# The tokens' factors computed earlier and with fewer steps, and expert products that wait for their weights piece by piece

## The reference

```
logits = x @ w_gate;  e_idx = argmax(logits, axis=1)
probs = exp(logits - logits.max(-1, keepdims=True))
probs /= probs.sum(-1, keepdims=True) + 1e-09
gate_w = probs[arange(N), e_idx]
eom = 1.0 / (1.0 + exp(-(x @ w_output_gate)))
for e in range(E):
    mask = e_idx == e
    h = maximum(x[mask] @ w1[e], 0.0)
    out[mask] = gate_w[mask, None] * eom[mask, e, None] * (h @ w2[e])
```

## Time and profile before

| | us |
|---|---|
| median of 3 runs | 1444.78 (1444.0 to 1448.49) |
| the profiled execution | 1446.43 |
| its span, first to last instruction | 1444.7 |
| busy: PE, DVE, ACT, POOL | 1358.1, 866.3, 621.3, 382.7 |

### The profile page before, as it was taken

The page is one execution under the profiler, slowest core; times in us unless marked ns, Lnnn a source line. Parts: engine busy times, 40 slices in busy tenths (PEclk is TensorE's granted clock), DMA queues, the critical chain, the costliest instruction groups (busy, mean ns, idle before and its releaser), DMA issues. The chain is left out here.

```text
span 1444.7 us, 24541 instructions
## 1 busy us (share of the span) xinstructions
PE 1358.1 (94%) x7653; PEld 1197.4 (83%) x7653; DVE 866.3 (60%) x1622; ACT 621.3 (43%) x1523; POOL 382.7 (26%) x307
## 2 busy tenths in 40 slices
PE   4999999999999999559979999989999999999998
PEld 3788888888888888447867888868999999999997
DVE  2899999999999998774434444436532323332232
ACT  3888888888888887311143011005411111111111
POOL 4122222222222235586498022023001010200000
PEclk9999999999999999769989999999999999999999
DMA  7755555556656664266366221016300000000000
GB/s 167 172 128 127 126 126 126 130 130 133 132 131 133 134 133 124 98 210 217 119 221 223 66 82 65 15 45 181 110 30 15 30 15 31 15 22 1 0 23 22
DMA packets 125343, 144.91 MB, mean 100 GB/s; under 512 B 48416, under 2 KB 91040, under 8 KB 123360
## 3 DMA queue, kind: packets, MB, share of 16 engines
q1 hardware_dynamic: 110192, 103.37, 29.2%
q10 hardware_dynamic: 11648, 29.36, 6.3%
q0 software_dynamic: 3440, 11.27, 2.7%
HBM read 84.48 MB, written 19.66 MB: 72 GB/s over the span
## 5 line engine op out<-in xcount | busy, mean ns | idle before, releaser
L637 ACT ACTIVATE p_hl<-ps_t 128x512 fp32r<-128x512 f32 (+1 forms) x336 | 196.0, 586 | 79.7 <-PE ps_t L812 77.5
L761 DVE TENSOR_TENSOR p_hl<-ps_t,p_hl 128x512 fp32r<-128x512 f32 (+1 forms) x336 | 217.4, 667 | 14.3 <-ACT p_hl L637 8.4
L893 PE MATMUL ps_o<-p_hl,v_hl 128*128 128x512 f32 x558 | 198.4, 436 | 0.0
L812 PE MATMUL ps_t<-ident,probs 128*128 128x128 f32 x1296 | 196.2, 273 | 0.8 <-DVE p_hl L761 0.4
L812 PEld LDWEIGHTS ps_t<-ident,probs 128*128 128x128 f32 x1296 | 160.0, 140 | 27.0 <-DVE p_hl L761 3.5
L653 ACT ACTIVATE probs<-ps_s_late,neg_max 128x384 f32<-128x384 f32 x288 | 165.2, 578 | 28.3 <-DVE neg_max L704 26.3
L1714 ACT ACTIVATE silu<-ps_g 128x384 f32<-128x384 f32 x72 | 35.4, 492 | 315.8 <-PE ps_g L1820 315.7
L927 PE MATMUL ps_s_late<-kq_t 128*128 128x384 f32 x640 | 159.8, 360 | 9.1 <-ACT probs L653 7.7
L1767 DVE TENSOR_TENSOR silu<-ps_g,silu 128x384 f32<-128x384 f32 x72 | 40.1, 558 | 212.0 <-ACT silu L1714 212.0
L1139 POOL TENSOR_TENSOR w_parts<-raw_w,w_parts 128x1024 fp32r<-128x1024 f32 x56 | 132.0, 2395 | 99.7 <-ACT w_parts L1207 99.7
L1207 ACT ACTIVATE w_parts<-raw_w 128x1024 fp32r<-128x1024 f32 x56 | 58.5, 1058 | 220.4 <-POOL w_parts L1139 97.7
(11 more groups left out here) (202 smaller groups left out, 2862.2 us busy)
## 6 DMA issues: line engine op xcount, KB each, us to landing
raw_w<-in_moe_w ACTq DMA_DIRECT2D x56, 512.0 KB, 4.1
kq_t<-kept_rows SPq DMA_DIRECT2D x30, 608.0 KB, 6.3
kq_t<-kept_rows SPq DMA_DIRECT2D x32, 320.0 KB, 7.1
raw_k<-in_k SPq DMA_DIRECT2D x32, 288.0 KB, 5.6
raw_v<-in_v SPq DMA_DIRECT2D x16, 576.0 KB, 4.8
kq_t<-kept_rows SPq DMA_DIRECT2D x30, 288.0 KB, 6.6
raw_q<-in_q SPq DMA_DIRECT2D x32, 256.0 KB, 4.1
y_by_slot<-x_out SPq DMA_DIRECT2D x25, 256.0 KB
```

Source lines behind the costliest of these rows:

```text
L637: nc.scalar.activation(p_hi[prob_ring(kind, m)][:, 0:w], T[ring(kind, j)][:, 0:w], ACT.Copy).then_inc(hi_ready, 1)
L761: nc.vector.tensor_tensor(p_lo[n][:, 0:w], t[:, 0:w], p_hi[n][:, 0:w].bitcast(F32), ALU.subtract).then_inc(t_free, 1)
L812: last = nc.tensor.transpose(dst[:, n * P:(n + 1) * P], src, ident[:, :])
L893: last = nc.tensor.matmul(sums_of(kind, what)[:, :], v_hl[v_par][:, c * P:(c + 1) * P], part[:, :], start=(i == 0 and n == 0), stop=(i == ...
```

## The change

Two edits, both in `route_and_experts`.

1. The chain of factors. The eleven DVE instructions become six. The numerator 1 is left out, and the two factors' denominators are multiplied before one reciprocal of 18 columns; of the 144-column operations one product and two reductions remain. The chain stands ahead of xs_parts(0) instead of behind it.
2. The waits for weights on PE. `up` waited for all four pieces of w1, then ran over the halves h and inside over the chunks c; now it runs over c, waits for piece c, and inside over h. `down` waited for all four pieces of w2; now it waits for one piece every two chunks. The matmuls are the same; both HB banks are filled in turn, and up_half is incremented for both at the last chunk.

```
+                dve.wait_ge(exp_out, 1)
+                link(nc.vector.tensor_tensor(big[2][:, :], big[3][:, :], onehot[:, :], ALU.mult))
+                nc.vector.reduce_sum(small[1][:, :], by_e(big[1]), AX)
+                link(nc.vector.reduce_sum(small[3][:, :], by_e(big[2]), AX))
+                link(nc.vector.tensor_scalar(small[3][:, :], small[3][:, :], 1.0, None, ALU.add))
+                link(nc.vector.scalar_tensor_tensor(out=small[2][:, :], in0=small[1][:, :], scalar=1e-9,
+                                                    in1=small[3][:, :], op0=ALU.add, op1=ALU.mult))
+                nc.vector.reciprocal(coef[:, :], small[2][:, :]).then_inc(coef_ready, 1)
+
                 xs_parts(0)
-
-                dve.wait_ge(exp_out, 1)
-                link(nc.vector.reduce_sum(small[1][:, :], by_e(big[1]), AX))
-                link(nc.vector.tensor_tensor(big[1][:, :], big[1][:, :], onehot[:, :], ALU.mult))
-                link(nc.vector.reduce_sum(small[0][:, :], by_e(big[1]), AX))
-                link(nc.vector.tensor_scalar(small[1][:, :], small[1][:, :], 1e-9, None, ALU.add))
-                link(nc.vector.reciprocal(small[2][:, :], small[1][:, :]))
-                link(nc.vector.tensor_scalar(big[3][:, :], big[3][:, :], 1.0, None, ALU.add))
-                link(nc.vector.reciprocal(big[2][:, :], big[3][:, :]))
-                link(nc.vector.tensor_tensor(big[2][:, :], big[2][:, :], onehot[:, :], ALU.mult))
-                link(nc.vector.reduce_sum(small[3][:, :], by_e(big[2]), AX))
-                link(nc.vector.tensor_tensor(small[0][:, :], small[0][:, :], small[2][:, :], ALU.mult))
-                nc.vector.tensor_tensor(coef[:, :], small[0][:, :], small[3][:, :], ALU.mult).then_inc(coef_ready, 1)
-
                 hidden(0)
...
-                    pe.wait_ge(w_ready[0], W1P * e + W1P)
                     pe.wait_ge(xst_ready, i + 1)
                     base = pe.snap((e % 2) * (2 * WCOLS))
-                    for h in range(FH):
-                        for c in range(DC):
+                    for c in range(DC):
+
+                        pe.wait_ge(w_ready[0], W1P * e + c + 1)
+                        for h in range(FH):
...
-                                                                    stop=(c == DC - 1))
-                        last.then_inc(up_half, 1)
+                                                    stop=(c == DC - 1))
+                            if c == DC - 1:
+                                last.then_inc(up_half, 1)
...
-                    pe.wait_ge(w_ready[1], W2P * e + W2P)
...
                     for c in range(FC):
+                        if c % (FC // W2P) == 0:
+
+                            pe.wait_ge(w_ready[1], W2P * e + c // (FC // W2P) + 1)
```

## The result

The changed kernel takes 1432.38 us (median, 1430.69 to 1434.58), beside 1444.88 for the kernel before on the same chip: a ratio of 0.9904, 95% interval 0.9884 to 0.9924, so 11 to 17 us less. The forecast was 1431, in a range of 1424 to 1437. The profiled execution took 1430.82 us, its span is 1429.0.

A forecast was written before the change was run, and what follows sets the result against it. From 775.9 us the kernel was taken as PE's row of matmuls, so only reaching that state earlier counts: 8.5 us (chain) plus 5.4 (pieces) is 13.9, giving 1431 us, range 1424 to 1437.

The forecast's parts named there:

- The chain, 12.6 us at tile 1: DVE before tile 0's parts: six instructions take 1.6 us in idle time, cost 0; tile 1 starts 12.6 us earlier.
- rival C: DVE's product meets POOL's residues in its new place, if started after 618.33: tile 1 7.5 us late, 1447 us; chance 0.04.
- the rest of a gather, 0.95 us: Chain in its new place beside POOL's gathers: the most that contention could cost, 0.95 us, still covered by idle time.
- What is late next: tile 0's store behind L1111: DVE's copy of tile 1 waits until 664.2 for a store in SP's queue; down(2) starts at 667.6, lead 10.1 us.
- G: Lead left after the store's wait and PE's low clock, carried through tile 5 to experts 4 and 5: 8.0 to 10.0, taken 8.5.
- delay up(3) by some 4 us inside this same wait: If DVE's nameless pause until 656.85 recurs, it delays tile 3's up product some 4 us within the store's wait, costing nothing else.
- ACT and POOL follow PE: Preparation of weights for experts 4 and 5 waits for tile 5's down product, so it moves earlier if tile 5 does.
- The pieces, 5.4 us: PE's up product at tile 9, waiting piece by piece, ends 4.7 to 5.9 us sooner; 5.4 taken.
- rival B: The pieces bring nothing, since PE's clock falls in the trickle and later waits eat the rest: 1436 us; chance 0.16.
- Two waits for the price of one: Tile 8's gain from the pieces, up to 6 us, does not add, because tile 9 waits for POOL again.
- 150 waits at nothing: Three more waits per up and per down product on PE, 150 in all, cost 0; other bound 16 us.
- The lock: DVE's two-SBUF-input product waits for all eight POOL residues, about 17 us, not one of 2.4 us as the skill page says.

The follow-up runs named there:

- e4: The changed kernel with the old long chain put ahead of tile 0's parts, moved but not shortened: 1447.89 us, ratio 1.0001 to the kernel before.
- e5: The changed kernel with the last tiles' rows saved from POOL's queue instead of SP's: 1423.44 us, ratio 0.9855 to the kernel before.
- e1: The kernel before with the new short chain ahead of tile 0's parts, PE's waits and loops as they were: 1440.66 us, ratio 0.9955.
- e8: The changed kernel itself, unaltered, run on the chip of e5 to e7: 1433.78 us, ratio 0.9929 to the kernel before.
- the first four experiments: e1 to e4, all on one chip, testing chain and pieces apart: ratios 0.9955, 0.9948, 1.0012 and 1.0001 to the kernel before.
- e2: The changed kernel with the old chain back behind tile 0's parts, so the waits by pieces alone: 1439.42 us, ratio 0.9948 to the kernel before.
- e7: The changed kernel with each of PE's waits for a piece issued four times, 600 waits more: 1433.35 us, ratio 0.9929 to the kernel before.
- e3: The kernel before with the new short chain left in the old place, behind tile 0's parts: 1449.83 us, ratio 1.0012.
- e11: e5 with weight preparation on ACT and POOL reordered, from expert 3 on, with expert 5's second weights ahead of expert 6's first: 1412.8 us, ratio 0.978.
- e6: e5 with eight of POOL's residues made between the gathers of kept rows and those of late rows: 1423.38 us, ratio 0.9855 to the kernel before.

## Why the prediction was right

*The chain, 12.6 us at tile 1.* Right: 12.8 us from t0. DVE's six instructions took 1.62 us where 1.6 stood, in idle time. Their safety was overrated: I put the point from which rival C decides at 618.33, 3.3 us after the chain's start, and reckoned contention only while a residue runs. In e4 a start 0.59 us before the first residue's row was already too late. Between the end of the last instruction with two SBUF inputs (L1385, 614.81) and POOL's residues (616.98) lie 2.2 us: that is the margin of this change, and a few instructions more would eat it. The bound from the other side, "the rest of a gather, 0.95 us", was not one.

*What is late next: tile 0's store behind L1111.* Right in place; right in size too, but by two errors that cancel, and with one thing that it passed over. DVE's wait at L1378 ended at 664.39 (forecast 664.2), down(2) began at 668.11 (667.6), L1111 was issued nearly when it was before (657.58):
```profile
657.36 0.37 SPq L1111 DMA_DIRECT2D x_of_last_tiles<-xs_late  x1
```
e5 shows it as the cause: with the saving out of SP's queue the copy no longer waits and 10.3 us more are won (1433.78 to 1423.44). The lead that was to remain, 8.5 us, measured 8.3 at tile 9 (e1) and 8.2 at tiles 3 to 7 of the changed kernel.

That agreement is in part luck. The sum was a lead of 10.1 us at down(2) less 1.6 for a low clock after PE's wait. Counted from t0, down(2) was to begin at 54.3 us and began at 56.1, a lead of 8.3; and the clock then took nothing (8.2 at tile 3 and still 8.2 at tile 7), since the low clock (0.56 from 656 to 662) came ahead of down(2) and not behind it. Where PE's idle time came as drawn, in e8, down(2) began at 55.3, a lead of 9.1, and the clock took 2.8, which left 6.3 us at tile 4 (76.5 - 70.2), below the 8.0 to 10.0 given for G; at tile 9 it was 11.9 (155.5 - 143.6) where 13.9 was forecast. (The trace of before is from another execution, not of e8's chip.) So the mechanism held on both chips, and the size of G hit only where the pause was there.

I had expected a pause of DVE to "delay up(3) by some 4 us inside this same wait" and to leave PE idle 5.7 us. In the changed kernel DVE paused 10.05 us and PE dripped one matmul in 1.4 to 2.1 us, so that up(3) ended at 667.76 rather than 661.5, just when the store let go: PE's idle time lay ahead of 656 and not behind 661.5. The idle 5.7 us as I drew them are e8's 7.67. After the first four experiments I doubted my step and held that pause and store bind together, so that e5 would win nothing; on e5's chip the pause was absent and the store alone was in the way. What e5 would win where the pause is there was not measured.

*ACT and POOL follow PE.* Right: ACT's first piece of expert 3's second weights came at 711.57, beside 721.16, still right behind tile 5's down, and the residues at 712.71, beside 722.30, 8.2 us earlier counted from t0.
```profile
711.57 1.06 ACT L1207 ACTIVATE w_parts<-raw_w 128x1024 fp32r<-128x1024 f32 x1 [11.04 <-PE ps_y L1504]
```

*The pieces, 5.4 us.* Right: 5.0 in e2, 5.5 in the difference of changed kernel and e1 at tile 9 (147.2 - 141.7). It ended 1.5 us after the fourth piece where 1.4 to 2.6 stood. What I had weighed against it, a falling clock in the trickle (rival B), did not come at tile 8 (1.00) and was slight at tile 9 (0.87 in its window, after the 3.92 us wait).

*Two waits for the price of one.* Tile 8's gain of about 6 us was said not to add, since tile 9 waits for POOL again: in the table e2 is 6.3 us ahead at tile 8 and 5.0 at tile 9.

*150 waits at nothing.* Right; 600 more cost nothing either (e7).

*The lock.* The Trainium skill's page "SBUF — State Buffer", section "Who interferes with whom", says that the loser blocks until the first instruction finishes. Four traces differ from it: the product was held through a row of eight residues each time, 17.19 (before), 17.20 (e2), 17.59 (e3) and 19.18 us (e4), and never let in between two. e2's row:
```profile
622.09 17.20 DVE L1384 TENSOR_TENSOR big<-big,onehot 128x144 f32<-128x144 f32 x1
```
By the page's price e3 would have lost at most one residue there, 2.4 us, and e4 would have been near the changed kernel; the measurement decides. An instruction with only one of its two inputs in SBUF was not held: in the changed kernel L1350, with the other in PSUM, took 0.69 us at 628.11, in the midst of the residues (616.98 to 635.76).

**What stays open.** The cause of DVE's pause (7.85 us before, 10.05 changed, 9.81 in e1, 11.26 in e2, 9.90 in e3; 4.90 in e4) and of PE's dripping beside it, which the trace of before hardly has (one gap of 1.01 us). It was in every trace of e1 to e4 (one chip) and in those of before and after, in none of e5 to e11 (three other chips), which speaks for something of the chip but does not show it. In all six traces the last of it ended 43.3 to 43.9 us from t0. Loading of instructions is a rival that nothing tested; the DMA views speak against it, since a transfer of the instruction queue (0.02 MB) stands at 647 us in the changed kernel and at 645 in e8, which has no pause, while e2 and e3 have the pause and none from 636 to 659. Nor did I test how long before the residues a product must start to escape; e4 gives one point (0.59 us, caught) and the changed kernel another (its last instruction with two SBUF inputs ended 2.2 us ahead, free).

## What to carry to other kernels

A wait that is taken away on the path is worth what the next late thing leaves of it: follow the queue of every engine that the early work now meets, DMA queues included, since a store behind someone else's waiting transfer cost 10 of 22 us here (e5). A preparation in a ring of pieces should be ordered by when each piece is due, and waited for piece by piece. A VectorE instruction with two SBUF inputs belongs well before a run of GpSimd arithmetic of the kind seen here (tensor_tensor, reading SBUF) or after it, never at its edge.

## What the runs showed of the hardware

- A DVE product with two SBUF inputs is held for the whole of a run of GpSimd tensor_tensors (17.2 to 19.2 us over eight, beside 0.31 to 0.34 alone), and was caught already when its row started 0.59 us before the first of them.
- A DVE tensor_tensor with one input in PSUM and one in SBUF is not held by them (0.69 us at 628.11, in the midst of eight).
- Waits on semaphores that are already satisfied cost PE nothing that shows: with 600 more, 841 matmuls in 175.00 us both times, and 1433.35 us beside 1433.78.
- PE fed in bursts of six matmuls with gaps of 0.65 to 0.92 us kept a granted clock of 1.00; one undivided idle of 7.67 us was followed by 0.62 in the next 7.9 us, so by the lower of the two levels (1.2 and 2.4 GHz) for most of them. Seven us in which PE was busy for 2.13 were followed by 0.56 in the next 6.
- Attention and routing were over at 610.6 to 615.6 us in thirteen profiled executions (by t0 in the table, with 611.75 in e6 and 611.55 in e7) of kernels that do not differ there, so effects of a few microseconds later on have to be counted from their end.
